# Two FF units at a time, with both layers' half-row matmuls side by side, in a two-layer fused MLP

## The reference

```python
w = softmax(weight, axis=-1)                      # 8 heads x 7 taps
x = causal_conv(x, w)                             # each feature by its head's 7 taps, along the sequence
h = x @ w_in1;  g = h / (1 + exp(-1.702 * h));  x = g @ w_out1         # 192 -> 2048 -> 192
h = x @ w_in2
P = a[0] + a[1]*h + a[2]*h**2 + a[3]*h**3
Q = 1 + |b[0]|*|h| + |b[1]|*h**2
out = (P / (Q + 1e-6)) @ w_out2                                       # 192 -> 2048 -> 192
```

## Time and profile before

| | |
|---|---|
| median of 3 runs | 1423.31 us (1422.83 to 1423.45) |
| the profiled execution | 1423.74 us |
| its span in the trace | 1421.6 us |
| TensorE busy | 1351.4 us, 95% |
| VectorE busy | 1300.1 us, 91% |
| ScalarE busy | 1070.3 us, 75% |
| GpSimd busy | 403.8 us, 28% |
| granted TensorE clock over the span | 0.992 of full |

### The profile page before, as it was taken

How to read it: one execution, slowest core, us unless ns; L and a number is a source line. 1 busy time by engine, 2 the same in 40 slices (tenths; PEclk the granted TensorE clock), 3 DMA queues, 4 the chain that set the end, 5 groups by cost and what they waited for, 6 DMA issues and landing times. The chain is left out here.

```text
span 1421.6 us, 18695 instructions
## 1 busy us (share of the span) xinstructions
PE 1351.4 (95%) x4896; PEld 752.5 (53%) x4896; DVE 1300.1 (91%) x1989; ACT 1070.3 (75%) x2025; POOL 403.8 (28%) x278
## 2 busy tenths in 40 slices
PE   3999999999999999999999999999999999999876
PEld 2455555555555555555555555555555555555432
DVE  5379999999999999999999999999999999998996
ACT  4377877778787877868777687777878788686885
POOL 4222232222222222222222223222222222232232
PEclk9999999999999999999999999999999999999997
DMA  8000000000000000000000000000000000000000
GB/s 222 19 12 1 12 12 1 23 1 11 11 11 11 0 22 0 11 11 0 22 0 11 11 11 11 0 22 0 11 11 11 11 0 11 0 1 12 0 12 11
DMA packets 32878, 20.28 MB, mean 14 GB/s; under 512 B 10321, under 2 KB 30801, under 8 KB 32849
## 3 DMA queue, kind: packets, MB, share of 16 engines
q1 hardware_dynamic: 32372, 19.93, 5.1%
q10 hardware_dynamic: 477, 0.01, 0.0%
HBM read 13.64 MB, written 6.29 MB: 14 GB/s over the span
## 5 line engine op out<-in xcount | busy, mean ns | idle before, releaser
L669 POOL TENSOR_TENSOR work<-work 128x512 f32<-128x512 f32 x256 | 381.2, 1489 | 970.0 <-ACT work L413 970.0
L256 PE MATMUL acc<-g,down 128*128 128x512 f32 x1024 | 491.5, 599 | 5.5 <-DVE g L579 5.3
L248 PE MATMUL h<-x_a_hi,up_a_hi 128*128 128x512 f32 x512 | 266.3, 520 | 55.1 <-DVE x_b L549 18.8
L428 ACT ACTIVATE work<-h 128x512 f32<-128x512 f32 x256 | 151.5, 592 | 200.1 <-PE h L252 200.1
L579 DVE SCALAR_TENSOR_TENSOR g<-work 128x512 f32<-128x512 f32 x256 | 286.3, 1118 | 0.1
L256 PEld LDWEIGHTS acc<-g,down 128*128 128x128 f32 x1024 | 188.3, 190 | 144.6 <-issue 112.4
L262 PE MATMUL acc<-g,down 128*64 128x512 f32 x1024 | 251.9, 609 | 0.0
L571 DVE SCALAR_TENSOR_TENSOR work<-work 128x512 f32<-128x512 f32 x256 | 207.8, 812 | 11.8 <-ACT work L405 11.2
L248 PEld LDWEIGHTS h<-x_a_hi,up_a_hi 128*128 128x128 f32 x512 | 96.2, 188 | 227.1 <-issue 164.5
L249 PE MATMUL h<-x_a_lo,up_a_hi 128*128 128x512 f32 x512 | 202.3, 395 | 0.0
L251 PE MATMUL h<-x_b,up_b_hi 128*128 128x512 f32 x512 | 202.2, 395 | 0.0
(11 more groups left out here) (75 smaller groups left out, 1066.3 us busy)
## 6 DMA issues: line engine op xcount, KB each, us to landing
out<-y_out SPq DMA_DIRECT2D x16, 384.0 KB, 2.5
x_in_a<-in_x SPq DMA_DIRECT2D x16, 256.0 KB, 2.8
down<-in_moe_w_out SPq DMA_DIRECT2D x8, 384.0 KB, 6.3
x_in_b<-in_x SPq DMA_DIRECT2D x32, 64.0 KB, 2.5
work<-in_moe_w_in SPq DMA_DIRECT2D x8, 256.0 KB, 5.8
work<-in_moe_w_in SPq DMA_DIRECT2D x16, 128.0 KB, 6.0
wts<-in_weight ACTq DMA_DIRECT2D x2, 0.4 KB
wts<-in_weight SPq DMA_DIRECT2D x2, 1.3 KB
```

What stands on the lines that cost most here:

```text
L248: mm(h, l.up_a_hi[:, cols], l.x_a_hi[:], start=True, stop=False)
L256: return mm(l.acc[:, 0, :], l.down[:, f, 0:P], l.g[:, f % G_SLOTS, :], start=f == 0, stop=f == STEPS - 1)
L669: tt(m[slot], sq[slot], seed, ALU.mult).then_inc(m_ready, 1)
```

## The change

The counter now runs over pairs of units, "duos": n = 8*i + s, eight steps in a tile, and an operation of ScalarE, VectorE and GpSimd in the layers' chains works on both units of a duo, 1024 columns. The two `h` banks of a layer now hold the two units of one duo. The order of each engine's step is new, and so are the lags, in duos: layer 1's activation in the step of its up product, down 1 one step later, layer 2's up product, t1, sq, ab, t2, t3, q, seed and z1 at lag 10, its m, s1, s2, z2 and g at lag 11, down 2 at lag 12.

The fifth matmul of a unit, with the low weights of part `b`, is now `up_rest`: it uses 64 of the 128 rows, which hold the high part of x; layer 1 has it in the lower and layer 2 in the upper half of the rows, and the two layers' are issued one after the other. The low weights of both layers share one tensor. The `b` parts of the down products are paired across the two layers, in the two halves of one PSUM bank `acc_b`, and no longer across two units, so that the two halves need no addition. Layer 1's result is copied and split straight from PSUM. The inputs of the up products have two buffers (index p), and the split of the next tile's input is now in step 7 of the tile before. The transposes have a PSUM bank of their own, `turned`. VectorE's `t2` waits for `h2_read`, the last of ScalarE's three reads of `h`; GpSimd multiplies into one buffer `m`. `CONV_AT` spreads the convolution's 21 operations as three in each of the steps 0 to 6 and none in step 7.

The core of the diff; where "..." stands, lines are left out, among them all removed lines of the functions shown above.

```diff
+DUOS = STEPS // 2
...
-LAG_ACT1 = 1
-LAG_DOWN1 = 2
-LAG_UP2 = 19
-LAG_P = 20
-LAG_RATIO = 21
-LAG_DOWN2 = 22
...
-S_X1 = 0
-S_ACC1 = 1
-S_X2 = 2
-S_XT = (4, 5)
-S_CONV = 5
-S_ACC2 = 5
...
+LAG_GELU = 0
+LAG_DOWN1 = 1
+LAG_UP2 = 10
+LAG_RATIO = 11
+LAG_DOWN2 = 12
...
+S_XT = (7, 0)
+S_X1 = 7
+S_X2 = 0
+S_ACC2 = 3
+S_YT = (5, 6)
...
+            l.acc_a = pb("acc_a" + n, [P, NT])
...
+        up_b_lo = sb("up_b_lo", [P, FF], F32R)
...
+        acc_b = pb("acc_b", [P, NT])
+        turned = pb("turned", [P, NT])
+        L1.lo_row, L1.acc_row = 0, DB
+        L2.lo_row, L2.acc_row = DB, 0
...
+        sqa, sqb, t1a, t1b, za, zb, ab, seed, m, s1, s2 = (work[:, k, :, :] for k in range(11))
...
+            def up(l, d, p):
...
+                for k in range(2):
+                    h, cols = l.h[:, k, :], slice((2 * d + k) * P, (2 * d + k + 1) * P)
+                    mm(h, l.up_a_hi[:, cols], l.x_a_hi[:, p, :], start=True, stop=False)
+                    mm(h, l.up_a_hi[:, cols], l.x_a_lo[:, p, :], start=False, stop=False)
+                    mm(h, l.up_a_lo[:, cols], l.x_a_hi[:, p, :], start=False, stop=False)
+                    mm(h, l.up_b_hi[:, cols], l.x_b[:, p, :], start=False, stop=False)
+            def up_rest(l, d, p, k):
+                f, rows = 2 * d + k, slice(l.lo_row, l.lo_row + DB)
+                return mm(l.h[:, k, :], up_b_lo[rows, f * P:(f + 1) * P], l.x_b[rows, p, :], start=False, stop=True)
...
+            def down_b(l, d, slot, k):
+                f = 2 * d + k
+                return mm(acc_b[l.acc_row:l.acc_row + DB, :], l.down[:, f, P:D], l.g[:, slot, k, :],
                           start=f == 0, stop=f == STEPS - 1)
...
+            def step(i, s, p):
+                n = i * DUOS + s
+                u, v1, v2 = n - LAG_UP2, n - LAG_DOWN1, n - LAG_DOWN2
+                d2, p2 = (s - LAG_UP2) % DUOS, (p + (s - LAG_UP2) // DUOS) % 2
...
+                if live(n):
...
+                    if s == 0:
+                        pe.wait_ge(x1_hi_done, 4 * (i + 1))
+                        pe.wait_ge(x1_lo_done, 3 * (i + 1))
+                    wait(pe, g1_ready, n)
+                    up(L1, s, p)
                 if live(u):
...
+                    if d2 == 0:
                         pe.wait_ge(x2_hi_done, 2 * i)
                         pe.wait_ge(x2_lo_done, 2 * i)
...
+                    wait(pe, t3_ready, u)
+                    up(L2, d2, p2)
+                for k in range(2):
+                    if live(n):
+                        last1 = up_rest(L1, s, p, k)
+                    if live(u):
+                        last2 = up_rest(L2, d2, p2, k)
+                if live(n):
+                    last1.then_inc(h1_ready, 1)
                 if live(u):
...
+                    last2.then_inc(h2_ready, 1)
+                e1, e2 = (s - LAG_DOWN1) % DUOS, (s - LAG_DOWN2) % DUOS
+                if live(v1):
+                    if isinstance(v1, int) and v1 < DUOS and e1 % 2 == 0:
+                        pe.wait_ge(down1_loaded[e1 // 2], 16)
+                    if e1 == 0:
+                        wait(pe, x2_hi_done, 2 * i)
+                        wait(pe, x2_lo_done, 2 * i)
+                    pe.wait_ge(g1_ready, v1 + 1)
+                if live(v2):
...
                         wait(pe, acc2_read, 2 * (i - 1))
...
+                    pe.wait_ge(g2_ready, v2 + 1)
+                for k in range(2):
+                    if live(v2):
+                        down_b(L2, e2, (s - LAG_DOWN2) % 2, k)
+                    if live(v1):
+                        down_b(L1, e1, (s - LAG_DOWN1) % 2, k)
+                if live(v1):
+                    down_a(L1, e1, (s - LAG_DOWN1) % 2).then_inc(g1_used, 1)
+                if live(v2):
+                    down_a(L2, e2, (s - LAG_DOWN2) % 2).then_inc(g2_used, 1)
...
+                wait(act, h1_ready, DUOS * (tile - 1))
+                fn(L1.x_a_hi[:, p, :], conv_a[:], ACT.Copy).then_inc(x1_hi_done, 1)
...
+                fn(L1.x_b[0:DB, p, HALF:NT], conv_b[DB:P, :], ACT.Copy).then_inc(x1_hi_done, 1)
...
+            def step(i, s, p):
+                n = i * DUOS + s
+                k, v, t = n - LAG_UP2, n - LAG_RATIO, i - 1
                 if live(k):
                     if isinstance(k, int) and k == 0:
...
+                        act.wait_ge(w2_lo, 2 * CHUNKS)
                     act.wait_ge(h2_ready, k + 1)
+                    wait(act, z1_ready, k - 1)
+                    fn(t1[(s - LAG_UP2) % 2], L2.h[:], ACT.Identity, scale=scale_a3, bias=par[:, 2:3])
                     wait(act, m_ready, k - 1)
...
+                    fn(sq[(s - LAG_UP2) % 2], L2.h[:], ACT.Square, scale=scale_root)
                     wait(act, q_ready, k)
...
+                    fn(ab, L2.h[:], ACT.Abs, scale=scale_b0).then_inc(h2_read, 1)
+                e = n - LAG_GELU
+                if live(e):
+                    act.wait_ge(h1_ready, e + 1)
+                    wait(act, g1_used, e - 1)
+                    fn(L1.g[:, (s - LAG_GELU) % 2, :, :], L1.h[:], ACT.Gelu_apprx_sigmoid).then_inc(g1_ready, 1)
+                if s == S_X2 and tile_live(t):
+                    act.wait_ge(g1_used, DUOS * i)
+                    wait(act, h2_ready, DUOS * (t - 1))
+                    fn(L2.x_b[DB:P, 1 - p, :], acc_b[DB:P, :], ACT.Copy).then_inc(x2_hi_done, 1)
+                    fn(L2.x_a_hi[:, 1 - p, :], L1.acc_a[:], ACT.Copy).then_inc(x2_hi_done, 1)
+                if s == S_ACC2 and tile_live(i - 2):
+                    act.wait_ge(g2_used, DUOS * (i - 1))
+                    wait(act, y_transposed, 2 * (i - 2))
+                    fn(y_b[0:DB, :], acc_b[0:DB, :], ACT.Copy).then_inc(acc2_read, 1)
+                    fn(y_a[:], L2.acc_a[:], ACT.Copy).then_inc(acc2_read, 1)
+                if turns(i, s):
+                    evacuate_x(*turns(i, s))
                 if s in S_YT and tile_live(i - 2):
                     half = S_YT.index(s)
                     act.wait_ge(y_transposed, 2 * (i - 2) + half + 1)
                     wait(act, y_stored, 16 * (i - 2))
                     fn(y_out[:, 2 * half:2 * half + 2, :],
...
+                       turned[:, 0:2 * D].rearrange("p (j d) -> p j d", d=D), ACT.Copy).then_inc(y_ready, 1)
+                if s == S_X1 and tile_live(i + 1):
+                    split_x1(i + 1, 1 - p)
+                if live(v):
+                    act.wait_ge(m_ready, v + 1)
+                    wait(act, z2_ready, v)
+                    fn(s1, m, ACT.Square, scale=root_c, bias=root_c * b1).then_inc(s1_ready, 1)
+                    wait(act, g2_ready, v)
+                    fn(s2, m, ACT.Square, bias=b2).then_inc(s2_ready, 1)
                 if live(k):
...
+                    act.wait_ge(q_ready, k + 1)
+                    wait(act, z1_ready, k)
+                    wait(act, m_ready, k)
+                    fn(seed.bitcast(I32), sq[(s - LAG_UP2) % 2].bitcast(I32), ACT.Copy, scale=-1.0, bias=SEED_BITS)\
+                        .then_inc(seed_ready, 1)
...
+            def step(i, s, p, conv, at):
+                n = i * DUOS + s
+                u, v, t = n - LAG_UP2, n - LAG_RATIO, i - 1
+                h, tu, sk, zu = L2.h[:], t1[(s - LAG_UP2) % 2], sq[(s - LAG_UP2) % 2], z[(s - LAG_UP2) % 2]
+                zv, gv = z[(s - LAG_RATIO) % 2], L2.g[:, (s - LAG_RATIO) % 2, :, :]
                 if live(u):
...
+                    dve.wait_ge(h2_read, u + 1)
                     tt(tu, tu, h, ALU.mult).then_inc(t2_ready, 1)
...
+                    dve.wait_ge(t2_ready, u + 1)
+                    stt(tu, tu, par[:, 1:2], h, ALU.add, ALU.mult).then_inc(t3_ready, 1)
+                    stt(sk, ab, 1.0 + 1e-6, sk, ALU.add, ALU.add).then_inc(q_ready, 1)
                 if live(v):
                     dve.wait_ge(s1_ready, v + 1)
                     dve.wait_ge(z1_ready, v + 1)
                     stt(zv, s1, scale_c * d1, zv, ALU.add, ALU.mult).then_inc(z2_ready, 1)
...
+                if s == S_X1 and tile_live(i + 1):
+                    split_x1(i + 1, 1 - p)
+                for op in conv[at[s]:at[s + 1]]:
+                    op().then_inc(conv_steps, 1)
                 if live(v):
                     dve.wait_ge(s2_ready, v + 1)
                     dve.wait_ge(z2_ready, v + 1)
...
+                    wait(dve, g2_used, v - 1)
                     stt(gv, s2, d2, zv, ALU.add, ALU.mult).then_inc(g2_ready, 1)
...
                 if live(u):
                     dve.wait_ge(seed_ready, u + 1)
                     dve.wait_ge(t3_ready, u + 1)
                     wait(dve, g2_ready, u - 1)
                     stt(zu, tu, par[:, 0:1], seed, ALU.add, ALU.mult).then_inc(z1_ready, 1)
...
+                if s == S_X2 and tile_live(t):
+                    dve.wait_ge(x2_hi_done, 2 * t + 1)
+                    tt(L2.x_b[0:DB, 1 - p, :], acc_b[DB:P, :], L2.x_b[DB:P, 1 - p, :].bitcast(F32), ALU.subtract)\
+                        .then_inc(x2_lo_done, 1)
```

(55 more changed lines are left out.)

341 lines of the change are left out of this document (99 added, 242 removed).

## The result

The changed kernel took **1802.29 us** (median of 4 runs, 1801.58 to 1803.55), the kernel before 1423.38 us beside it (4 runs, 1422.83 to 1424.45): ratio 1.2662, 95% interval 1.264 to 1.2684. Forecast were 1676 us and at most 1735. The direction was right, the size was not: of 379 us more the sum had 253.

What follows compares the result with a forecast made beforehand. TensorE bounded the kernel before; with VectorE's queue making it wait, 13 tiles of 100.8 us (1310) plus first and last stages gave a span of 1674, forecast 1676 us; own range 1620 to 1730, with rivals 1500 to 1735.

Steps and rivals of the forecast that it cites:

- the sum: Whole run: 93 + 73 + 1310 + 87 + 111 = 1674 us of span, forecast 1676 us, 253 us more than before.
- R0 to D1: Step 0 to 1: TensorE's downs wait for layer 1's split result, last in VectorE's queue, 14.29 us.
- D3 to D4: Step 3 to 4: ScalarE reads layer 2's result before s1, so g and TensorE's downs come late, 14.07 us.
- R7 to next R0: Step 7 to the next tile: ups wait for the split input on VectorE, 16.74 us; TensorE alone 9.97.
- The chain: Once round a tile along whatever comes last, R ending TensorE's ups, D starting its downs: 100.8 us against 83.9.
- The product's hold: GpSimd's product, started at q's end, holds VectorE's operation after z2 for 2.05 us per 1024 columns; bounds 0 and 2.56.
- the rule weighed there: Skill's lock-out of GpSimd and two-SBUF-input VectorE instructions: loss the product's whole 2.56 us, making the sum 1718.
- The operations of 1024 columns: ScalarE and VectorE operations priced from 256 and 512 columns: t2 starts at R + 3.17, released TensorE 0.23 us later.
- TensorE's duo without stops: TensorE's work for two units of both layers: 9.75 us in place of 10.13, four half-row matmuls taking 0.46.
- The rival of unpaired half rows: Half-row matmuls don't run together: 0.46 us more in four links, 1.9 a tile, 1704 us; chance 0.12.
- The order of waits: TensorE waits at steps 1, 3, 4, 6 and the tile's boundary, for 21 us of a tile.
- The rival that TensorE sets the pace: VectorE has the low parts ready before TensorE asks: 79.8 us a tile, 1382 us in all; chance 0.03.

Runs made afterwards that it cites:

- experiment 1: Changed kernel with GpSimd's product waiting for z1 in place of seed: 1590.94 us, ratio 1.1187.
- experiment 7: Changed kernel with product after z1, layer 2's downs a step later, layer 1's low parts behind q, convolution and x split a step earlier: 1406.31 us.
- experiment 12: Kernel of experiment 7 with the transposes of y issued behind the step's up matmuls: 1390.02 us, ratio 0.9775.
- (10): Kernel of experiment 7 with four full-row matmuls in place of the half-row ones, output not the reference's: 1430.28 us, ratio 1.0075.
- experiment 3: Changed kernel with GpSimd multiplying only 64 of the 1024 columns, output not the reference's: 1594.52 us, ratio 1.1215.

## Why the prediction was wrong in size

The links of a tile, R (ups done) and D (downs start) as in the prediction, each with its step's number; the last column is what low-clock matmuls cost in the tile shown above, each against its like at 2.4 GHz:

| link | predicted | measured | of it low clock |
|---|---|---|---|
| R0 to D1 | 14.29 | 14.70 | 0 |
| D1 to R2 | 9.75 | 11.22 | 1.39 |
| R2 to D3 | 12.41 | 12.38 | 0 |
| D3 to D4 | 14.07 | 15.60 | 1.54 |
| D4 to R5 | 10.32 | 12.66 | 1.74 + 0.47 |
| R5 to D6 | 13.07 | 13.05 | 0 |
| D6 to R7 | 10.19 | 11.63 | 1.36 |
| R7 to next R0 | 16.74 | 18.04 | 1.37 |
| tile | 100.8 | 109.28 | 7.9 |

- **The step that failed** is in "The chain": every link but the program's first matmuls was priced at the full-clock slots of the earlier trace rows, which come from a TensorE that hardly stops. The text had TensorE wait for 21 us of a tile in five stops, and took those stops as lost time only. Each also made the next matmuls slow, and these lie on the chain: 7.9 of the 8.5 us that a tile took beyond the sum. The 13 steady tiles, from R at 173.35 to R at 1593.22, took 1419.9 us for 1310, so 110 of the missing 126 us. The other 17 are in the first and the last stages (381 us for 364), where how much the clock took was not measured apart. The other 0.6 us of a tile is mostly the first link, 0.41 over. The row that could have warned was in the text: the first up product behind the long start took 0.77 for 0.50.
- **The product's hold** was right in size: 2.05 predicted, 2.05 measured in experiment 1. Its place was not quite the forecast one. The product comes later than the operation behind z2: in the tile shown it holds L560 (the third split), g, and the second convolution operation L528. All of these stand ahead of g's end, so the link pays the same. By the rule weighed there, a wait for the whole product, the hold would have been 2.37 us, the product's mean in experiment 1, where it holds nothing. The gap is smaller than it looks: the three held operations shown start 0.12 to 0.29 us after the product and are free again 0.14 to 0.20 us before its record ends.
- **The operations of 1024 columns** came as worked out: t2 starts R + 3.20 (719.91 to 723.11) for 3.17. A released TensorE starts 0.11 to 0.15 us behind the releaser's record (733.81 + 0.69 to 734.61 is one), for the 0.23 of the sum.
- **TensorE's duo without stops** takes 9.83 us for 9.75 (724.20 to 734.03 in experiment 7). The pairs do run side by side, but not at 0.46 for four: the first begins 0.09 late and the four take 0.66 with the change behind them. The rival of unpaired half rows is wrong.
- **The order of waits** was right at all five places. The boundary decides most: its stop was 6.36 us of the 4 to 7 given.
- **The rival that TensorE sets the pace** was right as a mechanism and wrong for this order. It gave 1382 us, with 79.8 a tile, for a kernel whose TensorE never waits. The four moves of experiment 7 and that of 12 bring such a kernel about, and it takes 1390, with 80.71 a tile.
- **The range** left out a cost that no term bounded: it reached to 1735 for half rows and a slightly longer hold, and no case had a lower clock.

Where did the change's gain go? TensorE's part of a tile fell, though by less than foretold (from 83.9 to 80.7 us in experiment 12, for 79.8), and the half rows are worth 24 us of it (10). It was lost in the order. VectorE's queue put the product's hold, g and the splits one behind the other, all after three reads of `h` by ScalarE, while TensorE had only its own step's work as cover.

## What to carry to other kernels

When a change makes the bounding engine wait, count the waits and then price the matmuls behind each at the lower clock: in the changed kernel a stop of 2.5 us cost another 1.4, a stop of 4.2 another 2.2. Take it as a likely cost, not as a sure one, since some stops of that length cost nothing in experiment 3. Batching operations in pairs nearly doubles the latency of a link (z2 from 0.60 to 1.13 us, start to start), so the consumer needs a step more of lag (`LAG_DOWN2`), and the results that the next stage waits for go ahead of the fillers in the queue. A GpSimd operation belongs beside VectorE operations that read PSUM. In experiment 1 a product begun at 747.70 lay beside L594, L597 and `t2`, which took 0.69, 0.69 and 1.22 us as they do without one. Moving it by one wait was worth 211 us where VectorE was on the path, and 45 us where TensorE set the pace.

## What the runs showed of the hardware

- A stop of 2.10 us could be enough for 1.2 GHz, and one of 2.77 us could pass without it. In the changed kernel all 49 stops of 2.48 us and more between 180 and 1250 us were followed by slow matmuls. At one place of experiment 1 a stop of 2.10 us was followed by `down_b` of 3.63 us, at the same place of experiment 3 one of 2.14 us by 1.94 us. Within experiment 3, at the same place of two tiles, stops of 2.77 us were followed by 3.68 us (at 750.42) and by 1.94 us (at 463.73). So the length of the stop alone doesn't decide. No stop of 1.57 us or less in the tiles looked at was followed by slow matmuls.
- GpSimd's product holds VectorE also in an operation with a single input of many columns: L528, 128x256, took 2.45 us beside a product and 0.35 in the kernel of 7 without one. A VectorE operation with one of its two inputs in PSUM was not held (L594 and L597 in experiment 1, 0.69 us).
- Half-row matmuls in two halves ran in pairs in either order of issue, with two of them starting within 0.02 us also as L1, L1, L2, L2. Why the order doesn't matter stays open.
